# Sums of two weight matrices in the attention loop: from 16 on ScalarE in a row to 8 on ScalarE and 8 on VectorE, one of each in five units

## The chip, the core and the metric

The kernel runs on one core of a Trainium2 chip. A core has five engines that run side by side, each its own instruction list in order: TensorE (PE, matrix products and transposes, with a weight load of its own, PEld), VectorE (DVE), ScalarE (ACT), GpSimd (POOL) and SyncE (SP, which here only starts transfers). They wait for each other by semaphores written out in the program. The metric is the device time of one execution in microseconds (us); lower is better.

## What is computed

```python
# q, k, v: (2, 8, 768, 64); n_global = 8, n_local = 96
scores = q @ k^T / 8 + bias            # bias falls with the distance, by head
keep   = (key < n_global) | (0 <= query - key < n_local)
a      = softmax(where(keep, scores, -1e9));  x = a @ v      # -> (1536, 512)
h      = x @ w_in                      # (512, 2048)
x2     = (h * tanh(softplus(h))) @ w_out                     # (2048, 512)
p      = domain_probs / sum            # (1536, 4)
y      = sum over 4 experts e of p[:, e] * (relu(x2 @ w1[e]) @ w2[e])
```

## The kernel before, in words

**Stages.** First the attention, for 16 heads (two batches of eight), then the product with w_in, its activation and the product with w_out (48 steps T), then four experts. The large products run in f16, with each f32 operand split into a high and a low part and three products of them. To split a matrix it is first scaled by a power of two found from a bound on its values. For w_in and w_out this bound is a maximum over partial sums of absolute values; the change is about these.

**The attention loop.** Heads go in pairs (PAIRS = 8). A pair has UNITS = 12 units: six tiles of 128 queries by two heads. So there are 96 units; unit n is pair n // 12, place n % 12. Only the keys of the band are taken: 128 at places 0 and 1, 256 at 2 and 3, 288 at the others. For a unit the work goes round between engines: PE makes scores (line 547, for two units at a time, at odd places, three units ahead), DVE adds the bias and finds the maximum (line 1120, two units ahead), ACT takes the exponential (line 850, two units ahead), PE transposes (line 579), ACT copies the high part of the result (line 891), DVE makes the low part (line 1231), PE multiplies with the values (line 598, two units behind). Three score buffers and two buffers of transposed weights tie these together. At places 0, 2, 4, 6 PE transposes q and k of the next pair into PSUM bank 3 (fill, line 502), which ACT copies out one place later (lines 840, 843). DVE divides and stores half a pair at places 8 to 10 and 1 to 3 (output, its large step, line 1160, at 10 and 3). In pair 0 ACT also sums three pieces of v (line 874, units 2, 4, 6) and DVE reduces others (line 1201).

**The sums.** w_in lies in the tile stage, w_out raw in wB, each in eight pieces of 128 x 1024. `weights_sum(n, c)` (line 861 on) is one ACT instruction that sums the absolute values of a piece into a column of wpieces. W_SUMS places them at the end of ACT's units 21 to 28 (w_in) and 33 to 40 (w_out). DVE's `weights_max(n)` (W_MAX, units 29 and 41) reduces the columns, PE's `share_max(n)` (W_SHARE, units 32 and 44) spreads the result over the partitions by a product into bank 3, and DVE's `matrix_scale` (line 1172, W_SCALE, units 34 and 46) reads it and makes the scale in four short instructions (lines 1060 to 1063), then releases w_scale (line 1174). As bank 3 is also that of the fills, the first fill of pairs 4 and 5 waits for w_scale.

**What the scales release.** POOL waits for w_scale 1, splits w_in in eight pieces of three instructions (lines 771, 774, 777), waits for w_scale 2, and splits w_out in the same way. SP starts the loads of the first experts' w1 and w2 into stage when w_in is split (w_split 1).

**The x turns.** X0_BANDED gives the units at which PE transposes one of four chunks of the finished output of pairs 0 to 3 (line 510, bank 3), ACT copies its high part at the next unit (line 928), and DVE makes the low part at the end of its unit after that (line 1216, x_ready): units 56, 68, 80, 87. PE's turn c waits for x_ready c. From place 9 of the last pair on (unit 93) PE also makes the first products with w_in (`EARLY`); the first waits for x_ready 4 and w_split 1.

**The next stage.** By step T: PE first product (line 608), ACT exponential (line 973), DVE lines 1347, 1349, 1353, ACT lines 989 and 991, DVE lines 1365, 1367, POOL line 816, ACT line 983, DVE line 1359, and six steps behind PE's product with w_out (line 677), which waits for w_split 2. From T = 6 on DVE reduces pieces of w1 and w2 (line 1070).

Of the kernel before, what the change touches and what calls it, by code (L numbers as in the profile page):

```python
# [36 lines left out]
def program(nc, q, k, v, n_global, n_local, w_in, w_out, probs, w1, w2, out):  # L37
# [13 lines left out]
    UNITS = 2 * QT  # L51
# [21 lines left out]
    with ExitStack() as ctx:  # L73
# [166 lines left out]
        w_piece, w_sum = sem("w_piece"), sem("w_sum")  # L240
        w_max = sem("w_max")
# [71 lines left out]
        X0_BANDED = [m * UNITS + 8 for m in range(PAIRS - 4, PAIRS - 1)] + [(PAIRS - 1) * UNITS + 3]  # L313
# [12 lines left out]
        W_SUMS = ({0: 21, 1: 33}, {0: UNITS})  # L326
        W_MAX = ({n: at + PIECES for n, at in W_SUMS[0].items()}, {0: UNITS + PIECES})
        W_SHARE = ({0: 2 * UNITS + 8, 1: 3 * UNITS + 8}, {0: UNITS + 9})
# [156 lines left out]
        def _(pe):  # L485
            def fill(i, slot, k, banded):
# [9 lines left out]
                if banded and k == 0 and isinstance(m, int):  # L496
                    if m in (4, 5):
                        pe.wait_ge(w_scale, m - 3)
                    if m >= PAIRS - 2:
                        pe.wait_ge(x_ready, m - PAIRS + 3)  # L500
# [331 lines left out]
        def _(act):  # L832
# [27 lines left out]
            def weights_sum(n, c):  # L860
# [3 lines left out]
                act.wait_ge(w_sum, PIECES * n + c + len(V_SUMS))  # L864
# [18 lines left out]
            def pair(i, slot, banded):  # L883
                for u in range(UNITS):
# [19 lines left out]
                    for n, start in W_SUMS[0 if banded else 1].items():  # L904
                        if at - start in range(PIECES):
                            if n and at == start:
                                act.wait_ge(w_max, n)
                            weights_sum(n, at - start)
# [6 lines left out]
                if not banded and not after(i, slot):  # L915
                    act.wait_ge(tables_free, 1)
                    load_w_out()
                    act.wait_ge(w_max, 1)
                    for c in range(PIECES):
                        weights_sum(1, c)  # L920
# [97 lines left out]
        def _(dve):  # L1018
# [53 lines left out]

            def weights_max(n):

                halves = 1 if n < 2 else 2
                if n < 2:
                    dve.wait_ge(w_sum, PIECES * (n + 1) + len(V_SUMS))
                else:
                    dve.wait_ge(w_piece, PIECES * (n - 1))
                dve.tensor_reduce(wpart[:, 0:halves], wpieces[:].rearrange("p (h c) -> p h c", h=halves),  # L1080
# [95 lines left out]
            def matrix_step(m, u, banded):  # L1176


                at, case = m * UNITS + u, 0 if banded else 1
                for n, col in ((0, SC_WIN), (1, SC_WOUT)):  # L1180
# [254 lines left out]
            with dve.Else():  # L1435
                full_tables(chain(table_step))
                attention(False)
                dve.sem_inc(tables_free, 1)
                weights_max(1)
# [26 lines left out]
```

## Time and profile before

| | us |
|---|---|
| median of 3 runs | 910.69 (910.62 to 911.55) |
| the profiled execution | 911.57 |
| its span in the profile | 909.7 |
| attention, first to last line 1231 | 16.2 to 150.0 |

The profile counts from the start of the span. An engine is busy while one of its instructions runs; register, branch and semaphore instructions don't count. Matmuls are pipelined and their ends are modelled. A row of the timeline gives start and length, and in brackets how long the engine was idle before and which instruction released it. A row of busy times by stretch gives, behind the stretch and its length, the busy time of each engine in it with the number of its instructions, and then the clock that was granted to TensorE as a part of 2.4 GHz.

### The profile page before, as it was taken

How to read it: one execution, taken by the hardware profiler on the slowest of the kernel's cores; microseconds unless marked ns; L12 is line 12 of the kernel's file. 1: busy time of each engine (PE TensorE's matmuls, PEld its weight loads, DVE VectorE, ACT ScalarE, POOL GpSimd, SP SyncE). 2: the span in 40 equal slices, each digit the busy share in tenths (PEclk: the TensorE clock that was granted, in tenths of full speed). 3: DMA queues.
4: the chain of work that ended last, by engine and by line, in shares of the span. 5: the costliest groups of instructions: out<-in, count | busy, mean ns of one | idle time of the engine just before them, and what ended most of it. 6: DMA issues, size and time to landing. Idle time of an engine off the chain costs nothing.

```text
span 909.7 us, 12637 instructions
## 1 busy us (share of the span) xinstructions
PE 874.2 (96%) x4916; PEld 443.7 (49%) x4916; DVE 501.0 (55%) x1010; ACT 316.3 (35%) x597; POOL 263.6 (29%) x218
## 2 busy tenths in 40 slices
PE   6878999899999999999999999999999999999998
PEld 6666776444444444444444444444444444444443
DVE  7665887999999999984641224322134322212121
ACT  4798886544554555463020111101020101101020
POOL 1368993222222232220009400068000193000000
PEclk9898999999999999999999999999999999999999
DMA  9771320000000000202000400000400000000001
GB/s 222 244 251 39 124 99 1 1 1 1 1 7 3 1 1 1 93 3 93 4 6 0 180 6 1 6 0 8 177 1 2 4 0 0 1 24 23 35 12 49
DMA packets 52004, 39.19 MB, mean 43 GB/s; under 512 B 40816, under 2 KB 41712, under 8 KB 51440
## 3 DMA queue, kind: packets, MB, share of 16 engines
q1 hardware_dynamic: 49888, 34.31, 12.6%
q10 hardware_dynamic: 2064, 4.19, 1.3%
q8 instruction: 31, 0.51, 0.2%
q14 instruction: 21, 0.17, 0.1%
HBM read 35.35 MB, written 3.15 MB: 42 GB/s over the span
## 4 chain that ended last, share of the span: by engine, by line
PE 70%; DVE 20%; ACT 7%; issue 2%; POOL 0%; DVEq 0%; ACTq 0%
PE bank L608 58%; PE bank L677 5%; DVE tmp L1349 4%; DVE tmp L1367 3%; DVE xT L1365 3%; PE bank L547 2%; DVE tmp L1347 2%; PE bank L579 2%; ACT scaled L866 2%; DVE tmp L1353 2%; PE bank L598 2%; DVE hid L1359 1%; ACT tmp L989 1%; ACT tmp L850 1%; ACT tmp L891 1%
## 5 line engine op out<-in xcount | busy, mean ns | idle before, releaser
L962 ACT ACTIVATE hid<-bank 128x512 f16<-128x512 f32 x96 | 57.2, 596 | 413.8 <-PE bank L608 413.8
L608 PE MATMUL bank<-xT,wA 128*128 128x512 f16 (+1 forms) x864 | 194.6, 379 | 0.0
L1340 DVE SCALAR_TENSOR_TENSOR hid<-bank,hid 128x512 f16<-128x512 f32 x96 | 66.3, 691 | 177.2 <-ACT hid L962 177.2
L677 PE MATMUL bank<-hid,wB 128*128 128x512 f16 x576 | 133.8, 383 | 5.4 <-ACT acc L946 4.2
L608 PEld LDWEIGHTS bank<-xT,wA 128*128 128x128 f16 x864 | 84.5, 98 | 100.7 <-issue 0.2
L608 PE MATMUL bank<-wA,hid 128*128 128x512 f16 x576 | 125.3, 379 | 0.0
L608 PE MATMUL bank<-wB,hid 128*128 128x512 f16 x576 | 125.3, 379 | 0.0
L608 PE MATMUL bank<-xT,wB 128*128 x576 | 125.3, 379 | 0.0
L816 POOL TENSOR_TENSOR tmp<-tmp 128x512 f32<-128x512 f32 x48 | 67.8, 1412 | 195.8 <-DVE tmp L1367 195.8
L771 POOL TENSOR_SCALAR stage<-stage,sc 128x1024 f32<-128x1024 f32 x32 | 35.8, 1120 | 255.1 <-DVEq L1333 245.3
L1418 DVE SCALAR_TENSOR_TENSOR acc<-bank,pg,acc 128x512 f32<-128x512 f32 x36 | 27.0, 751 | 131.7 <-PE bank L608 131.7
L677 PEld LDWEIGHTS bank<-hid,wB 128*128 128x128 f16 x576 | 56.6, 99 | 75.2 <-DVE hid L1359 5.2
L608 PEld LDWEIGHTS bank<-wB,hid 128*128 128x128 f16 x576 | 56.4, 98 | 68.0
L608 PEld LDWEIGHTS bank<-xT,wB 128*128 128x128 f16 x576 | 56.4, 98 | 68.0
L608 PEld LDWEIGHTS bank<-wA,hid 128*128 128x128 f16 x576 | 56.3, 98 | 68.0
L983 ACT ACTIVATE hid<-tmp 128x512 f16<-128x512 f32 x48 | 30.3, 630 | 116.5 <-POOL tmp L816 116.5
L1231 DVE SCALAR_TENSOR_TENSOR tmp<-bank,tmp 128x384 f16<-128x384 f32 (+2 forms) x96 | 47.0, 490 | 34.2 <-ACT tmp L891 33.1
L608 PE MATMUL bank<-xT,hid 128*128 (+1 forms) x288 | 63.6, 379 | 0.0
L579 PE MATMUL bank<-ident,tmp 128*128 128x128 f32 x240 | 45.7, 290 | 8.7 <-DVE tmp L1231 6.6
L850 ACT ACTIVATE tmp<-tmp 128x288 f32<-128x288 f32 (+2 forms) x96 | 48.6, 507 | 15.5 <-DVE tmp L1120 14.4
L1349 DVE SCALAR_TENSOR_TENSOR tmp<-tmp 128x512 f32<-128x512 f32 x48 | 52.1, 1086 | 1.6
L608 PEld LDWEIGHTS bank<-xT,hid 128*128 128x128 f16 x288 | 28.2, 98 | 34.0
(111 smaller groups left out, 940.8 us busy)
## 6 DMA issues: line engine op xcount, KB each, us to landing
stage<-in_moe_w SPq DMA_DIRECT2D x8, 2048.0 KB, 9.9
stage<-in_moe_w_in SPq DMA_DIRECT2D x1, 4096.0 KB, 14.5
wB<-in_moe_w_out ACTq DMA_DIRECT2D x1, 4096.0 KB, 15.9
hid<-in_q SPq DMA_DIRECT2D x16, 192.0 KB, 3.3
hid<-in_k SPq DMA_DIRECT2D x16, 192.0 KB, 3.4
xT<-in_v SPq DMA_DIRECT2D x8, 384.0 KB, 4.9
out_y<-acc SPq DMA_DIRECT2D x12, 256.0 KB, 2.0
rows<-max SPq DMA_DIRECT2D x4, 128.0 KB, 3.8
```

The source lines that it names most:

```text
L579: last = pe.transpose(dst[:, b * P:(b + 1) * P], src[:, b * P:(b + 1) * P], ident[:])
L608: last = pe.matmul(dst, lhs(c, a), rhs(c, b), start=(c == 0 and n == 0), stop=(c == chunks - 1 and n == 2))
L677: last = pe.matmul(psum(4 + d), w_out_s[:, a, f // 2, f % 2, d * P:(d + 1) * P], hv[:, T % RING, b, :], start=(f == 0 and n == 0), stop=(f ...
L771: pool.tensor_scalar(tmp, src, scale, 1.0, ALU.mult, ALU.mult).then_inc(w_part, 1)
L816: pool.tensor_tensor(g_t[T % 4], g_t[T % 4], r_t[T % 2], ALU.mult).then_inc(g_ready, 1)
L850: act.activation(t, t, ACT.Exp, bias=nmax[:, u:u + 1], scale=-1.0).then_inc(p_ready, 1)
L962: act.activation(hv[:, f, 0, :], psum(f % 4), ACT.Relu).then_inc(f_hi, 1)
L983: act.activation(hv[:, m % RING, 0, :], g_t[m % 4], ACT.Copy).then_inc(h_hi, 1)
L1231: dve.scalar_tensor_tensor(pt[:, 1], src, P_SCALE, pt[:, 0], ALU.mult, ALU.subtract).then_inc(pT_dve, 1)
L1340: dve.scalar_tensor_tensor(hv[:, f, 1, :], psum(f % 4), 0.0, hv[:, f, 0, :], ALU.max, ALU.subtract).then_inc(f_ready, 1)
L1349: dve.scalar_tensor_tensor(n, u, 2.0, u, ALU.add, ALU.mult).then_inc(n_ready, 1)
L1365: dve.scalar_tensor_tensor(e_t, n, 2.0, r, ALU.add, ALU.mult).then_inc(e_ready, 1)
```

## The change

The pieces are dealt out: pieces 0 to 3 of each matrix to ACT (`BY_ACT`), 4 to 7 to DVE (`BY_DVE`), by a new function `weights_part_sum`, one tensor_reduce for the maximum of the absolute values of a piece into a column of wpieces. ACT's stand at the ends of units 22, 27, 32, 37 (w_in) and 46, 51, 56, 61 (w_out), DVE's in units 24, 29, 34, 39 and 48, 53, 58, 63. ACT's first sum of w_out now waits for the maximum over those of w_in, DVE's too. The maxima are taken in units 43 and 67, shared in 44 and 68, the scales made in 46 and 70. Fills of pairs 5 and 7 wait for w_scale. The x turns move to units 80, 85, 88, 90; the fills' waits for x_ready go. The branch for a mask that is no band changes in the same way; it isn't run with these inputs.

```diff
@@ -310,7 +311,7 @@
-        X0_BANDED = [m * UNITS + 8 for m in range(PAIRS - 4, PAIRS - 1)] + [(PAIRS - 1) * UNITS + 3]
+        X0_BANDED = [(PAIRS - 2) * UNITS + 8] + [(PAIRS - 1) * UNITS + u for u in (1, 4, 6)]
@@ -323,9 +324,13 @@
-        W_SUMS = ({0: 21, 1: 33}, {0: UNITS})
-        W_MAX = ({n: at + PIECES for n, at in W_SUMS[0].items()}, {0: UNITS + PIECES})
-        W_SHARE = ({0: 2 * UNITS + 8, 1: 3 * UNITS + 8}, {0: UNITS + 9})
+        BY_ACT, BY_DVE = range(4), [(4,), (5,), (6,), (7,)]
+        PARTS = len(BY_ACT) + len(BY_DVE)
+        W_ACT = ([2 * UNITS - 2 + 5 * c for c in BY_ACT], [4 * UNITS - 2 + 5 * c for c in BY_ACT])
+        W_DVE = ([2 * UNITS + 5 * c for c in range(len(BY_DVE))], [4 * UNITS + 5 * c for c in range(len(BY_DVE))])
+        W_ACT_FULL, W_DVE_FULL = ([UNITS + c for c in BY_ACT], [UNITS + c for c in range(len(BY_DVE))])
+        W_MAX = ({0: 3 * UNITS + 7, 1: 5 * UNITS + 7}, {0: UNITS + 8})
+        W_SHARE = ({0: 3 * UNITS + 8, 1: 5 * UNITS + 8}, {0: UNITS + 9})
@@ -494,10 +499,8 @@
-                    if m in (4, 5):
-                        pe.wait_ge(w_scale, m - 3)
-                    if m >= PAIRS - 2:
-                        pe.wait_ge(x_ready, m - PAIRS + 3)
+                    if m in (5, 7):
+                        pe.wait_ge(w_scale, (m - 3) // 2)
@@ -861,7 +864,9 @@
                 if c == 0:
                     act.wait_ge(w_out_loaded if n else w_loaded, 16)
-                act.wait_ge(w_sum, PIECES * n + c + len(V_SUMS))
+                    if n:
+                        act.wait_ge(w_max, n)
+                act.wait_ge(w_sum, len(BY_ACT) * n + c + len(V_SUMS))
@@ -1070,14 +1073,26 @@
+            def weights_part_sum(n, c):
+
+                if c == 0:
+                    dve.wait_ge(w_out_loaded if n else w_loaded, 16)
+                    if n:
+                        dve.wait_ge(w_max, n)
+                src = w_out_raw if n else stage
+                m, at = BY_DVE[c][0], len(BY_ACT) + c
+                dve.tensor_reduce(wpieces[:, at:at + 1], src[:, m * PIECE:(m + 1) * PIECE], AX_X, ALU.max,
+                                  apply_absolute_value=True).then_inc(w_part_sum, 1)
+
             def weights_max(n):
 
-                halves = 1 if n < 2 else 2
                 if n < 2:
-                    dve.wait_ge(w_sum, PIECES * (n + 1) + len(V_SUMS))
-                else:
-                    dve.wait_ge(w_piece, PIECES * (n - 1))
+                    dve.wait_ge(w_sum, len(BY_ACT) * (n + 1) + len(V_SUMS))
+                    dve.wait_ge(w_part_sum, len(BY_DVE) * (n + 1))
+                    dve.tensor_reduce(wpart[:, 0:1], wpieces[:, 0:PARTS], AX_X, ALU.max).then_inc(w_max, 1)
+                    return
@@ -1177,6 +1192,10 @@
                 at, case = m * UNITS + u, 0 if banded else 1
+                for n in range(2 if banded else 1):
+                    units = W_DVE[n] if banded else W_DVE_FULL
+                    if at in units:
+                        weights_part_sum(n, units.index(at))
```

## Rows read from the trace of the kernel before

**Rows 1.** Page, part 1: busy us (share of the span) and instructions of each engine.
```profile
PE 874.2 (96%) x4916; PEld 443.7 (49%) x4916; DVE 501.0 (55%) x1010; ACT 316.3 (35%) x597; POOL 263.6 (29%) x218
```

**Rows 2.** Busy time by stretch: stretch, its length, busy us by engine, granted clock, DMA.
```profile
core 0: us, PE busy (x) PEld busy (x) DVE busy (x) ACT busy (x) POOL busy (x), PEclk, DMA share, GB/s
47.93:84.71 36.78, 27.28 (x299) 21.99 (x298) 20.32 (x83) 35.44 (x82) 25.27 (x29) 0.91 0.45 138
88.11:113.84 25.73, 24.00 (x309) 19.92 (x306) 20.88 (x83) 20.85 (x51) 24.60 (x19) 1.00 0.40 122
```

**Rows 3.** Line 1231: instructions, ns min/median/max, first and last start us.
```profile
L1231 DVE SCALAR_TENSOR_TENSOR tmp<-bank,tmp x96: 275/556/559, 16.2 to 150.0; 128x384 f16<-128x384 f32 x64, 128x128 f16<-128x128 f32 x16, 128x256 f16<-128x256 f32 x16
```

**Rows 4.** Busy time by stretch: units 46, 10, 68-69, 44-45, 70.
```profile
89.27:91.60 2.33, 2.15 (x28) 1.46 (x27) 2.04 (x8) 0.63 (x2) 2.16 (x3) 1.00 0.07 15
33.24:34.38 1.14, 0.92 (x4) 0.54 (x4) 1.14 (x7) 0.78 (x2) 0.00 (x0) 0.50 0.92 374
116.31:118.78 2.47, 2.47 (x35) 2.00 (x35) 1.83 (x9) 2.31 (x6) 2.30 (x3) 1.00 1.05 402
87.19:89.27 2.08, 2.08 (x32) 1.64 (x30) 1.75 (x9) 1.92 (x5) 2.08 (x2) 1.00 1.04 232
118.78:120.52 1.74, 1.27 (x23) 0.83 (x22) 1.74 (x6) 0.63 (x2) 1.71 (x1) 1.00 0.45 159
```

**Rows 5.** Lines 866, 874 (ACT), 1201, 1070 (DVE): ns min/median/max, first and last start.
```profile
L866 ACT ACTIVATE scaled<-stage x8: 1042/1057/1096, 48.5 to 61.4; 128x1024 f32<-128x1024 f32 x8
...
L874 ACT ACTIVATE scaled<-xT x3: 827/830/831, 18.7 to 25.7; 128x768 f32<-128x768 f32 x3
...
L1201 DVE TENSOR_REDUCE vpart<-xT x4: 941/943/952, 14.2 to 23.9; 128x1 f32<-128x768 f32 x4
...
L1070 DVE TENSOR_REDUCE wpieces<-stage x32: 1208/1210/1220, 185.3 to 695.7; 128x1 f32<-128x1024 f32 x32
```

**Rows 6.** Busy time by stretch: units 1-6, 61-66, then 11-13 and 47-49.
```profile
16.70:27.04 10.34, 9.02 (x95) 7.71 (x95) 7.53 (x24) 8.93 (x22) 0.00 (x0) 0.83 0.98 223
107.79:114.79 7.00, 6.98 (x90) 6.00 (x86) 5.76 (x21) 6.73 (x15) 6.56 (x6) 1.00 0.91 341
34.38:39.93 5.55, 5.55 (x53) 4.67 (x52) 2.44 (x12) 2.73 (x8) 1.47 (x2) 0.57 1.01 411
91.60:94.69 3.09, 2.13 (x26) 1.82 (x26) 2.42 (x13) 2.63 (x8) 3.07 (x2) 1.00 0.02 5
```

**Rows 7.** Timeline of pair 7, PE, ACT, DVE: start us, length us, instruction.
```profile
141.24 0.52 PE L579 MATMUL bank<-ident,tmp 128*128 128x128 f32 x3
...
142.34 0.52 PE L579 MATMUL bank<-ident,tmp 128*128 128x128 f32 x3 [0.31 <-DVE tmp L1231]
...
144.38 0.52 PE L579 MATMUL bank<-ident,tmp 128*128 128x128 f32 x3
...
145.37 1.46 PE L608 MATMUL bank<-xT,wA 128*128 128x512 f16 x6
...
141.12 0.49 ACT L891 ACTIVATE tmp<-bank 128x384 f16<-128x384 f32 x1
...
142.11 0.68 DVE L1216 TENSOR_TENSOR xT<-bank,xT 128x512 f16<-128x512 f32 x1
```

**Rows 8.** Releases after the scales (line 1174), and POOL's last piece, from the timeline.
```profile
L1174 DVEq EVENT_SEMAPHORE  x2: 21/21/21, 71.2 to 90.8; - x2
...
141.19 2.14 POOL L777 TENSOR_TENSOR wB<-scaled,wB 128x1024 f16<-128x1024 f32 x1
```

**Rows 9.** Next stage: timeline of lines 1347, 816, 1349; then lines 1349, 677.
```profile
153.61 0.43 DVE L1347 TENSOR_SCALAR tmp<-tmp 128x512 f32<-128x512 f32 x1 [0.81 <-ACT tmp L973]
...
164.78 1.38 POOL L816 TENSOR_TENSOR tmp<-tmp 128x512 f32<-128x512 f32 x1 [4.83 <-DVE tmp L1367]
...
165.07 1.64 DVE L1349 SCALAR_TENSOR_TENSOR tmp<-tmp 128x512 f32<-128x512 f32 x1
...
L1349 DVE SCALAR_TENSOR_TENSOR tmp<-tmp x48: 691/693/1644, 154.1 to 395.4; 128x512 f32<-128x512 f32 x48
...
L677 PE MATMUL bank<-hid,wB x576: 376/379/634, 172.0 to 424.1; 128*128 128x512 f16 x192
```

More of the change, by code:

```diff
@@ L240, in program @@
         w_piece, w_sum = sem("w_piece"), sem("w_sum")
+        w_part_sum = sem("w_part_sum")
         w_max = sem("w_max")
@@ L903, in pair @@
                         load_w_out()
[L904 to L908, printed above, removed]
+                    for n in range(2 if banded else 1):
+                        units = W_ACT[n] if banded else W_ACT_FULL
+                        if at in units:
+                            weights_sum(n, units.index(at))
                     if at + 1 in V_SUMS:
@@ L917, in pair @@
                     load_w_out()
-                    act.wait_ge(w_max, 1)
-                    for c in range(PIECES):
+                    for c in BY_ACT:
                         weights_sum(1, c)
@@ L1071, in weights_part @@
                                   apply_absolute_value=True).then_inc(w_piece, 1)
+            def weights_part_sum(n, c):
[7 more added lines that the diff above has]
+                                  apply_absolute_value=True).then_inc(w_part_sum, 1)
             def weights_max(n):
-                halves = 1 if n < 2 else 2
                 if n < 2:
-                    dve.wait_ge(w_sum, PIECES * (n + 1) + len(V_SUMS))
-                else:
-                    dve.wait_ge(w_piece, PIECES * (n - 1))
-                dve.tensor_reduce(wpart[:, 0:halves], wpieces[:].rearrange("p (h c) -> p h c", h=halves),
+                    dve.wait_ge(w_sum, len(BY_ACT) * (n + 1) + len(V_SUMS))
+                    dve.wait_ge(w_part_sum, len(BY_DVE) * (n + 1))
+                    dve.tensor_reduce(wpart[:, 0:1], wpieces[:, 0:PARTS], AX_X, ALU.max).then_inc(w_max, 1)
+                    return
+                dve.wait_ge(w_piece, PIECES * (n - 1))
+                dve.tensor_reduce(wpart[:, 0:2], wpieces[:].rearrange("p (h c) -> p h c", h=2),
                                   AX_X, ALU.max).then_inc(w_max, 1)
@@ L1179, in matrix_step @@
                 at, case = m * UNITS + u, 0 if banded else 1
+                for n in range(2 if banded else 1):
+                    units = W_DVE[n] if banded else W_DVE_FULL
+                    if at in units:
+                        weights_part_sum(n, units.index(at))
                 for n, col in ((0, SC_WIN), (1, SC_WOUT)):
@@ L1438, in _ @@
                 dve.sem_inc(tables_free, 1)
+                for c in range(len(BY_DVE)):
+                    weights_part_sum(1, c)
                 weights_max(1)
```

## The prediction

> **What bounds the kernel now.** I read the head of the page first [rows 1]: TensorE (PE) is busy 96% of the 909.7 us span, VectorE (DVE) 55%, ScalarE (ACT) 35%. That is an average. The change touches only the banded attention, some 17% of the span, and there the busy shares by stretch are what counts [rows 2]. I cut this stage at the starts of the DVE instruction of line 1231, which runs once in each of the 96 units, in order [rows 3]; so a unit's length is the distance between two of them. "Unit 46" is pair 3, place 10.
>
> Two stretches with the same places in them (place 9 of one pair to place 6 of the pair after next, 21 units) are to be set side by side [rows 2]. Units 21 to 41, in which ACT makes all 16 sums of the weights, take 36.78 us: ACT is busy 35.44 of them, PE 27.28. Units 45 to 65 take 25.73 us with PE busy 24.00, DVE and ACT 20.9 each. So ACT bounds the loop while it sums; without the sums PE does, with DVE and ACT about 19% idle. A loop of short steps handed from PE to ACT to DVE and back can use little of that idleness at one time: this is the question of the whole case.
>
> **What is removed.** Units 45 to 65 hold one scale and one x turn, which I price by single units [rows 4]. The scale: unit 46 took 2.33 us, unit 10, at the same place and with the same work in the loop, 1.14; so 1.19 (unit 10 ran at the low clock, so rather more). The x turn: units 68 and 69 took 2.47, units 44 and 45 took 2.08, and unit 70 took 1.74 against 1.14; so 0.39 + 0.60 = 0.99. Without both the 21 units take 25.73 - 1.19 - 0.99 = 23.55 us. The 16 sums of before, with the scale of |w_in| that fell among them (unit 34) and was mostly hidden, therefore cost 36.78 - 23.55 = 13.2 us, 0.8 each against the 1.04 to 1.06 that one takes on ACT [rows 5]. All of this goes.
>
> **What is added: eight sums on ACT and eight on DVE.** On DVE no such sum stands in the attention. The same instruction on 1024 columns takes 1.21 us later in the kernel, and one on 768 columns takes 0.94 us in pair 0; ACT's on 768 takes 0.83 [rows 5]. From below: in 21 units DVE has 25.73 - 20.88 = 4.85 us free, 1.15 in five units, and ACT 1.16. Both sums would then fit, and cost 0 to 0.3 us for both (below nothing is excluded, since both engines only get more work). From above: each passes on whole, 1.04 + 1.21 = 2.25 us. In between lies the one place where the two kinds alternate: units 1 to 6 hold three ACT and three DVE sums of 768 columns and took 10.34 us, against 7.00 for the same places in units 61 to 66 [rows 6]. That is 3.34 us for three pairs, 1.11 for a pair that occupies 0.83 + 0.94 us, so 0.63 per us of work; for 2.25 us it gives 1.4. The clock was down for a part of it and the sums stood closer than five units apart, both of which make it high; the DVE sums at places 3 and 10 now sit beside the output step, where the scale, a few short DVE instructions, cost 1.19, which makes it low. I take 1.3. Eight pairs: 8 x 1.3 = 10.4 us (0 to 18.0).
>
> **The scales.** The scale of |w_in| moves from unit 34, where ACT hid most of it, to unit 46; that of |w_out| from 46 to 70. Each now stands in the open: 2 x 1.19, where before one was inside the 13.2. The one at 46 was in the time before already, so +1.2 us more.
>
> **The x turns.** There are four before and after, now at units 80, 85, 88 and 90 in place of 56, 68, 80 and 87: 4 x 0.99 either way. But turn 3 (unit 90) waits for the low half of turn 2, which DVE makes only at the end of its unit 90, and the first product in unit 93 waits for the low half of turn 3, at the end of DVE's unit 92. PE is in order: behind the wait are turn 91, the scores and the values. By the rows of pair 7 [rows 7]: the transposes of unit 90 start at 141.24 and end at 141.76, then come ACT's copy (0.49), line 1231 (0.56), line 1216 (0.68) and the steps between, to about 143.6, and 0.3 of transposes; unit 91's transposes start at 143.9 and not at 142.34, 1.6 later, of which 1.0 is in the price of a turn. At unit 93 the same chain runs from 144.90 to about 146.8, where the first product started at 145.37: 1.4 later, of which 0.6 is priced. Together +1.4 us (0 if PE's other waits cover it, 3.0 if nothing of it is in the price of a turn).
>
> The two waits of PE for x_ready at fills of pairs 6 and 7 go; they waited for nothing (no row). The wait of ACT for w_max at unit 46 stands three units behind its release: nothing.
>
> **GpSimd (POOL), behind both scales.** It splits |w_in| from the first scale on: released at 71.2, its last piece of w_out starts at 141.19 and takes 2.14 [rows 8], so it ends at 143.3, 72.1 us after the release, and is never idle between. The second scale came at 90.8, long before POOL wanted it, which is at half way, 36 us on. Now it comes at unit 70. From unit 46 to 70 it was 118.78 - 89.27 = 29.5 us [rows 4]; less two x turns (2.0) and with four pairs of sums (5.2) that is 32.7, still before POOL is ready for it. So POOL ends 72.1 us after the scale of unit 46. The first DVE instruction of the next stage, line 1347, started at 153.61 [rows 9], 62.8 us after that same point of before (90.8). Now this distance grows by four pairs of sums (5.2), the second scale (1.2) and the x turns' waits (1.4) to 70.6. POOL's last piece would thus run 1.5 us into the next stage. What this costs is shown by line 1349: 1.64 us when it starts behind a POOL tensor_tensor at 164.78, where its median is 0.69 and POOL's instruction takes 1.38 [rows 9]. So DVE's lines 1347 and 1349 wait for POOL, and they are where the chain runs (ACT and PE wait for their result). I take +1.5 us (0 to 2.1). The products with w_out start only at 172.0 [rows 9]; POOL ends at about 155, so PE doesn't wait for it. The loads of w1 and w2 start behind w_in's split, 11.6 us later; the first reader of them stands at 185.3 [rows 5], so nothing.
>
> The Trainium skill ("SBUF — State Buffer", "Who interferes with whom") says that DVE with two SBUF inputs, or in a two-port mode, blocks against GpSimd for whole instructions, and that tensor_reduce never does. The trace agrees: 1.64 against 0.69 us for the one, 1208 to 1220 ns in all 32 cases for the other. By the rule the new DVE sums don't slow down beside POOL's splits, and the tail above is real.
>
> **The sum.** -13.2 + 10.4 + 1.2 + 1.4 + 1.5 = +1.3 us. Against the profiled execution (911.57 us, with 909.7 of span) that is 912.9; against the median of 910.69, **912.0 us**. What comes behind the attention is the same work in the same order, so the difference is handed through whole.
>
> **The rivals.**
> Rival A, the sums are absorbed. With the idle 19% of DVE and ACT used, a pair costs 0 to 0.3. For it: the busy shares, and that ACT and DVE are loaded in turn, not one engine in every unit. Against it: units 1 to 6. Then the scale of unit 46 comes at 90.8 - 13.2 + 1.0 = 78.6; POOL ends 72.1 later, at 150.7, and the next stage would begin 62.8 + 1.0 + 1.2 + 1.4 = 66.4 later, at 145.0. If DVE's first lines wait for POOL to the last, the end comes 2.9 us earlier than before, if never, 8.6: 902.1 to 907.8, and as each wait is for one POOL instruction of three, about the middle, 905.5 us. Faster.
> Rival B, every sum is passed on whole (2.25 a pair), since a unit is a ring of PE, ACT and DVE with two buffers. For it: DVE's 0.68 us of line 1216 made unit 70 0.60 longer. Against it: 0.8 each even where ACT was the bound. -13.2 + 18.0 + 1.2 + 1.4 + 0 (POOL is done by then) = +7.4: 918.1 us. Slower; it decides from 1.4 us a pair on.
> Rival C, the clock. Among ACT's 16 sums the granted clock fell from 2.4 to 1.2 GHz for a while (mean 0.91 [rows 2]), behind a stretch in which PE was busy for 27.28 of 36.78 us; there it was covered, as ACT was the bound. In the open it isn't: units 11 to 13, up to unit 14, took 5.55 us at a mean of 0.57, units 47 to 49, up to unit 50, which are the same places, 3.09 at 1.00 [rows 6]. The sums now stand in the open with PE idle beside them, so one such spell costs 2.5 on top of the sum: 914.5 us. Slower.
> Rival D, the waits of the x turns and of POOL's tail aren't there: -13.2 + 10.4 + 1.2 = -1.6: 909.1 us, no difference to speak of. That the change doesn't do what it says can hardly be: the banded branch is the one in the trace.
>
> **How the numbers follow.** About 0.2%, 1.8 us, is what a measurement of this kernel can tell from no change, so "same" is 908.9 to 912.5. The sum as worked has 0.45; its terms move it by 1.5 either way, and a part of 0.12 lies above 912.5. Rival A 0.25, B 0.13, C 0.13, D 0.04. Faster 0.25; same 0.33 + 0.04 = 0.37; slower 0.12 + 0.13 + 0.13 = 0.38. The range leaves out the lower part of A and what lies past B: 904.5 to 918.0; the forecast alone is 910.5 to 913.5.
>
> **What would show it.** In the profile after: the distance of line 1231 over units 21 to 45 falls by about 8 us; single units with an ACT sum are 0.5 to 0.8 longer, with a DVE sum 0.5 at places 0 and 5 and about 1.1 at 3 and 10; PE waits for line 1216 ahead of unit 91 and ahead of the first product; POOL's last piece ends behind the first line 1347, which takes over 1 us. The forecast is wrong if the units with sums are no longer than their neighbours (A), if each is 1 us longer (B), or if the clock is low between units 22 and 66 (C).

## The result, and the profile after

The changed kernel takes 914.2 us (median of 7 runs, 912.56 to 914.89) against 910.62 for the kernel before (7 runs, 909.53 to 911.56): ratio 1.0039, 95% interval 1.0029 to 1.0049. Measured again, unaltered, on another chip it took 913.93 against 911.33: 1.0031 (1.0022 to 1.0041). So it is slower by 0.3 to 0.4%, about 3 us. The time forecast was 912.0, in a range of 904.5 to 918.0; the side on which it came out had a chance of 0.38.

The head of the page after: the span, the busy shares (as [rows 1]), and the granted clock in 40 slices.

```profile
span 912.3 us, 12632 instructions
...
PE 873.6 (96%) x4916; PEld 443.0 (49%) x4916; DVE 510.5 (56%) x1018; ACT 308.5 (34%) x581; POOL 263.8 (29%) x218
...
PEclk8899999999999999999999999999999999999999
```

The shares of the whole span say nothing: PE is at 96% as before. So I cut the attention as in the forecast, at the starts of the DVE instruction that makes the low part (line 1231 before, 1250 after). The stretches are units 21 to 45, 46 to 83, 84 to 92, 93 and 94, and from unit 95 to the next stage's first tensor_scalar (line 1347 before, 1366 after). Columns are those of [rows 2]: stretch, length, busy us of PE, PEld, DVE, ACT, POOL, clock, DMA. First the kernel after:

```profile
47.15:81.22 34.07, 28.40 (x361) 23.29 (x359) 27.08 (x95) 27.87 (x67) 12.27 (x18) 1.00 0.59 174
81.22:132.36 51.14, 42.94 (x547) 35.23 (x546) 41.63 (x148) 40.50 (x97) 47.30 (x34) 1.00 0.30 99
132.36:146.44 14.08, 10.03 (x123) 8.42 (x124) 10.01 (x35) 8.99 (x21) 13.27 (x10) 1.00 0.01 2
146.44:150.80 4.36, 4.36 (x40) 2.69 (x39) 1.68 (x6) 1.52 (x3) 4.09 (x4) 1.00 0.02 4
150.80:155.95 5.15, 5.15 (x57) 3.69 (x56) 3.20 (x6) 0.72 (x2) 3.96 (x3) 1.00 0.00 0
```

and the same five stretches of the kernel before, which [rows 2] cut elsewhere:

```profile
47.93:89.27 41.34, 31.84 (x363) 25.84 (x361) 23.93 (x98) 39.57 (x91) 29.66 (x32) 0.92 0.48 141
89.27:135.68 46.41, 42.93 (x553) 35.55 (x552) 37.98 (x140) 37.76 (x91) 44.02 (x32) 1.00 0.33 110
135.68:146.38 10.70, 9.68 (x118) 8.07 (x118) 8.80 (x35) 8.05 (x19) 7.29 (x5) 1.00 0.01 3
146.38:149.96 3.58, 3.58 (x37) 2.30 (x35) 1.67 (x7) 1.52 (x3) 0.00 (x0) 1.00 0.00 0
149.96:153.61 3.65, 3.65 (x46) 2.55 (x45) 1.70 (x7) 0.72 (x2) 0.00 (x0) 1.00 0.00 0
```

| stretch | before | after | difference |
|---|---|---|---|
| up to unit 21 | 47.93 | 47.15 | -0.78 |
| units 21 to 45 | 41.34 | 34.07 | -7.27 |
| units 46 to 83 | 46.41 | 51.14 | +4.73 |
| units 84 to 92 | 10.70 | 14.08 | +3.38 |
| units 93, 94 | 3.58 | 4.36 | +0.78 |
| unit 95 to the next stage | 3.65 | 5.15 | +1.50 |
| the rest of the span | 756.09 | 756.35 | +0.26 |
| sum, the span | 909.7 | 912.3 | +2.6 |

The first line is not the change: nothing is altered up there, and 0.70 of the 0.78 us lie ahead of the first unit. Nor is the last but one: the 48 steps of the next stage start at the same distances in both (the last at 241.39 us behind the first, and at 241.37), and the 0.26 comes behind them. The five lines between are the change: it costs 3.1 us, where the medians show 3.6 and 2.6. Outside stretches of low clock the length of a unit repeats from one execution to the next to some 0.02 us, so these differences are far sharper than the medians.

**Single units with a sum.** Kernel after, busy time by stretch: units 22 (an ACT sum, place 10), 24 (DVE, place 0), 27 (ACT, 3), 29 (DVE, 5) and 34 (DVE, 10).

```profile
48.21:49.91 1.70, 1.70 (x27) 1.24 (x26) 1.23 (x4) 1.70 (x5) 1.49 (x4) 1.00 1.03 324
50.73:52.40 1.67, 1.63 (x23) 1.42 (x22) 1.67 (x7) 0.67 (x2) 1.59 (x2) 1.00 1.08 383
54.98:57.30 2.32, 2.32 (x31) 2.04 (x27) 1.26 (x4) 2.32 (x6) 2.16 (x4) 1.00 1.08 388
58.15:60.12 1.97, 1.42 (x17) 1.04 (x16) 1.97 (x7) 1.28 (x3) 1.89 (x2) 1.00 0.57 134
65.14:67.41 2.27, 2.27 (x30) 1.57 (x30) 2.27 (x6) 0.89 (x2) 0.00 (x0) 1.00 0.06 13
```

The same places without a sum took 1.14 (place 10, [rows 4]), 0.82, 1.44, 1.43 and 1.14 us in the kernel before. So the sums cost 0.56, 0.85, 0.88, 0.54 and 1.13 us in their own units. In the units with a DVE sum DVE is busy for the whole of the unit and ACT for a good third to two thirds of it; in those with an ACT sum ACT is busy for the whole and DVE for half to three quarters. Over all 25 units (which take 28.11 us without a sum: the 23.55 us of the forecast's 21 units, and 4.56 for units 42 to 45) the four pairs cost 34.07 - 28.11 = 5.96 us, 1.49 a pair. In units 46 to 83 two x turns (2.0) went and a scale (1.2) came; 4.73 + 2.0 - 1.2 = 5.5, 1.38 a pair.

**The x turns.** Timeline of PE in the kernel after: the transposes of turns 2 and 3 (line 513) and the first product with w_in (line 611).

```profile
137.69 0.66 PE L513 MATMUL bank<-ident,acc 128*128 128x128 f32 x4 [1.31 <-DVE xT L1235]
...
141.87 0.66 PE L513 MATMUL bank<-ident,acc 128*128 128x128 f32 x4 [1.50 <-DVE xT L1235]
...
146.21 1.04 PE L611 MATMUL bank<-xT,wA 128*128 128x512 f16 x4 [1.20 <-DVE xT L1235]
```

In brackets stands PE's idle time before each: 1.31, 1.50 and 1.20 us, ended each time by DVE's line 1235 (1216 before), which makes the low half of the turn ahead. The transposes of unit 91 waited 0.31 us in [rows 7], for another line, and the first product not at all.

**POOL's tail.** Kernel after: the releases behind the two scales (line 1189, as 1174 in [rows 8]), POOL's last instruction of w_out, then the next stage's first DVE instructions.

```profile
L1189 DVEq EVENT_SEMAPHORE  x2: 21/21/21, 82.8 to 116.4; - x2
...
152.80 2.13 POOL L780 TENSOR_TENSOR wB<-scaled,wB 128x1024 f16<-128x1024 f32 x1
...
153.30 1.65 DVE L1334 TENSOR_TENSOR sc<-sc 128x1 f32<-128x1 f32 x1
154.98 0.16 DVE L1335 TENSOR_TENSOR sc<-sc 128x1 f32<-128x1 f32 x1
155.95 0.43 DVE L1366 TENSOR_SCALAR tmp<-tmp 128x512 f32<-128x512 f32 x1 [0.81 <-ACT tmp L976]
```

POOL is released at 82.8 and ends at 154.93, 72.1 us later, as in the kernel before. Line 1334 is a product of two columns of 128x1. The one like it in the kernel before took 0.15 us; here it starts 0.50 us behind the start of POOL's tensor_tensor and ends 0.02 us behind its end, 1.65 us long. All of the 1.50 us by which the stretch from unit 95 on grew are in this one instruction. The first tensor_scalar of the stage starts at 155.95, 1.0 us behind POOL's end.

### The profile page after: what moved, and what is told of

It is laid out like the page before. It is cut to its first block, busy times and chain, and to the rows that moved or that the text cites. A ratio compares the mean times of both kernels' runs of the same rounds, so it can differ in the third digit from the quotient of the medians.

```text
span 912.3 us, 12632 instructions
## 1 busy us (share of the span) xinstructions
PE 873.6 (96%) x4916; PEld 443.0 (49%) x4916; DVE 510.5 (56%) x1018; ACT 308.5 (34%) x581; POOL 263.8 (29%) x218
## 4 chain that ended last, share of the span: by engine, by line
PE 68%; DVE 22%; ACT 6%; issue 2%; SPq 1%; DMA 0%; POOL 0%; DVEq 0%; ACTq 0%
PE bank L611 58%; PE bank L680 5%; DVE tmp L1368 4%; DVE tmp L1386 3%; DVE xT L1384 3%; DVE tmp L1366 2%; PE bank L550 2%; DVE tmp L1372 2%; PE bank L582 1%; DVE hid L1378 1%; ACT tmp L896 1%; ACT tmp L992 1%; PE bank L601 1%; ACT tmp L853 1%; DVE tmp L1135 1%
## 5 line engine op out<-in xcount | busy, mean ns | idle before, releaser
L1250 DVE SCALAR_TENSOR_TENSOR tmp<-bank,tmp 128x384 f16<-128x384 f32 (+2 forms) x96 | 47.0, 489 | 28.4 <-ACT tmp L896 27.4
L896 ACT ACTIVATE tmp<-bank 128x384 f16<-128x384 f32 (+2 forms) x96 | 41.4, 431 | 11.1 <-PE bank L582 10.4
```

The costliest lines, as they stand in the source:

```text
L896: act.activation(pt[:, 0], src, ACT.Copy, scale=P_SCALE).then_inc(pT_act, 1)
L1250: dve.scalar_tensor_tensor(pt[:, 1], src, P_SCALE, pt[:, 0], ALU.mult, ALU.subtract).then_inc(pT_dve, 1)
```

## The experiments

Ratios are to the kernel before on the same chip; where I say what a run has gained on the changed kernel "by the ratios", the changed kernel stands at 1.0035, the mean of its two. With a clock that falls at different moments, the median of a dozen runs is good to about 1 us (of the version in 9 there are only six and five); where a trace has the answer to 0.1 us, I go by the trace and give the median beside it.

**1. x turns that don't wait for each other.**

```diff
-        X0_BANDED = [(PAIRS - 2) * UNITS + 8] + [(PAIRS - 1) * UNITS + u for u in (1, 4, 6)]
+        X0_BANDED = [4 * UNITS + 8, 6 * UNITS + 8, 7 * UNITS, 7 * UNITS + 4]
...
                         pe.wait_ge(w_scale, (m - 3) // 2)
+                    if m == 6:
+                        pe.wait_ge(x_ready, 1)
```

> The changed kernel with the x turns at units 56, 80, 84 and 88, so that no turn and no first product waits for the low half of the turn before. Theory 1 (the loss comes from PE's three waits for line 1235 in pair 7, 2.2 us beyond the price of the turns, and from POOL's tail, which ends 72.05 us after the first scale whatever the loop does): the waits go and the last unit of the loop comes 2.2 us earlier, but POOL still ends at about 154.9, so DVE's first instructions of the next stage wait for POOL 1.5 to 3 us and most of the gain is given back: 912.5 to 914 us, against 914.2 for the changed kernel. Theory 2 (PE's waits cost, POOL's tail does not): 912.0. Theory 3 (it is the sums alone, the waits are covered): 914.2.

Measured: 911.62 us, ratio 1.0012 (0.9998 to 1.0025), 2.1 us under the changed kernel by the ratios. Busy time by stretch: units 84 to 92, 93 and 94, and from unit 95 to the next stage.

```profile
137.68:148.21 10.53, 9.73 (x118) 7.97 (x119) 9.24 (x36) 8.45 (x20) 9.91 (x8) 1.00 0.01 2
148.21:151.90 3.69, 3.69 (x37) 2.37 (x36) 1.67 (x6) 1.52 (x3) 3.42 (x4) 1.00 0.02 4
151.90:155.96 4.06, 4.06 (x50) 2.96 (x49) 2.10 (x7) 0.72 (x2) 3.87 (x3) 1.00 0.00 0
```

Units 84 to 92 take 10.53 us against 14.08, units 93 and 94 3.69 against 4.36: 4.2 us less, of which 1.1 came back as the turn at units 57 and 58 of this kernel, so 3.1 us. That is more than the 2.2 that I had set down as waits. The units around the two turns at 84 and 88 take 10.53 us, less than in the kernel before with one turn, at 87 (10.70): in pair 7, where there are no fills, a turn that nothing waits for seems to cost less than the 1.0 among the fills, though no run has pair 7 without a turn.

POOL took a part of this back. Its last instruction, and DVE's small product and first scalar_tensor_tensor of the next stage:

```profile
156.16 2.21 POOL L782 TENSOR_TENSOR wB<-scaled,wB 128x1024 f16<-128x1024 f32 x1
...
154.40 0.55 DVE L1336 TENSOR_TENSOR sc<-sc 128x1 f32<-128x1 f32 x1
156.42 2.50 DVE L1370 SCALAR_TENSOR_TENSOR tmp<-tmp 128x512 f32<-128x512 f32 x1
```

POOL ends at 158.37, 2.4 us into the next stage. The small product took 0.40 us longer than in the kernel before (0.15), and the scalar_tensor_tensor 1.81 longer than the 0.69 that it takes in the changed kernel; the second step of the stage starts 3.60 us behind the first in place of 1.80. So POOL's tail costs 2.2 us here against 1.5, and 2.4 of the 3.1 us are left, near the 2.1 of the ratios. Theory 1, by which most of the gain would be given back, was wrong in size: about a quarter was.

**2. POOL shorter.** The first of the eight pieces of w_out is set to zero in place of being split.

```diff
                 hi, lo = (wB[:, (2 * c + s) * PIECE:(2 * c + s + 1) * PIECE] for s in range(2))
+                if c == 0:
+                    pool.memset(wB[:, 0:2 * PIECE], 0.0).then_inc(w_out_part, 1)
+                    continue
```

> The changed kernel with the first of the eight pieces of w_out not split by POOL but set to zero by one memset (this part of w_out is left out of the result), so that POOL ends about 3.5 us earlier; nothing else is touched. Theory 1: the 1.65 us of line 1334 (128x1, waiting for POOL's last tensor_tensor) fall back to 0.15, and the kernel takes 914.2 - 1.5 = 912.7 us. Theory 2 and 3 (POOL's tail is covered): 914.2, with line 1334 short and the time lost elsewhere.

Measured: 912.15 us, ratio 1.0014 (1.0001 to 1.0027). Timeline of POOL's last instruction and of the small product:

```profile
150.05 2.13 POOL L780 TENSOR_TENSOR wB<-scaled,wB 128x1024 f16<-128x1024 f32 x1
...
153.39 0.15 DVE L1337 TENSOR_TENSOR sc<-sc 128x1 f32<-128x1 f32 x1
```

POOL ends at 152.18, ahead of it, and the product takes 0.15 us. Unit 95 to the next stage is 3.65 us again, as in the kernel before: exactly the 1.50 are gone. Units 84 to 94 stayed as long as in the changed kernel (18.4 us). Theory 1 holds for this term, to 0.1 us in the trace; the ratios give 1.9 us.

**3. Both.** The two edits together.

> Both at once: x turns at 56, 80, 84, 88 and POOL's first piece of w_out left out (set to zero). Theory 1: the two losses add up once POOL is out of the way: 914.2 - 2.2 - 1.5 = 910.5 us, so that the turns apart are worth 2.2 us here and much less in the run where POOL stays long. Theory 2: 912.0. Theory 3: 914.2.

Measured: 911.55 us, ratio 1.0019 (1.0007 to 1.0032). By the medians this is a miss: no faster than either alone. In the trace the span was 907.4, units 84 to 92 took 10.53 and 93 and 94 3.70 us, as in run 1. But the loop was now so much shorter that the small product met POOL all the same (1.95 us long, a tail of 1.8 us), so this run did not take the tail away, and says nothing on whether the two add up. Its single runs went from 909.25 to 915.7, over 6.4 us; only run 1 (6.3) and the second measurement of run 4 (6.4) spread as far. More on this stands at the end, under the clock.

**4. The kernel before with the late turns.** Run twice.

```diff
-        X0_BANDED = [m * UNITS + 8 for m in range(PAIRS - 4, PAIRS - 1)] + [(PAIRS - 1) * UNITS + 3]
+        X0_BANDED = [(PAIRS - 2) * UNITS + 8] + [(PAIRS - 1) * UNITS + u for u in (1, 4, 6)]
...
-                    if m >= PAIRS - 2:
-                        pe.wait_ge(x_ready, m - PAIRS + 3)
```

> The kernel before with only the x turns moved to units 80, 85, 88 and 90; sums, scales and POOL as before (POOL ends some 10 us ahead of the next stage). Theory 1 and 2: PE waits for the low halves ahead of turns 2 and 3 and ahead of the first product, +2.2 us: 910.6 + 2.2 = 912.8 us. Theory 3: 910.6.

> The kernel before with only the x turns moved to 80, 85, 88 and 90, once more. Its trace showed the units 84 to 93 longer by 3.37 us (two more turns at 1.0 each and 1.4 of waits) and unit 93 by 0.78, so 2.1 us net, while its median was only 0.3 us above the kernel before, with 4.8 us less of low clock in its runs on average. If the 2.1 us are real and the clock hid them by chance: 911.5 to 912.9 here. If the later turns make the clock fall less often, which gives them back: the median stays within 0.8 us of the kernel before and the mean time at the low clock is again about 5 us shorter.

Measured: 910.61 us, 1.0003 (0.9994 to 1.0013), and again 911.62 us, 1.0011 (0.9997 to 1.0025). Busy time by stretch of the second, as in run 1:

```profile
132.46:146.53 14.07, 10.02 (x123) 8.42 (x123) 10.01 (x35) 8.97 (x21) 9.28 (x7) 1.00 0.00 1
146.53:150.89 4.36, 4.36 (x40) 2.69 (x39) 1.68 (x6) 1.51 (x3) 0.00 (x0) 1.00 0.01 4
150.89:154.54 3.65, 3.65 (x46) 2.55 (x45) 1.69 (x6) 0.72 (x2) 0.00 (x0) 1.00 0.00 0
```

Units 84 to 92 take 14.07 us and units 93 and 94 4.36, in both executions, the lengths of the changed kernel to 0.01; the last stretch is 3.65, since POOL is done. From unit 21 to the next stage both traces show 107.7 us against 105.7 before: +2.0. So the waits are made by the places of the turns alone. The medians show less, 0.3 and 1.0 us. The traces show where the rest may be. Behind the attention, too, both executions were shorter than the kernel before, by 1.70 us each, and it is all in one place: a group of 48 products with w_out. Busy time by stretch from the start of the 385th of them to that of the 433rd, kernel before and then the first of these two:

```profile
342.34:364.74 22.40, 22.40 (x96) 9.83 (x97) 21.65 (x29) 12.72 (x22) 6.56 (x5) 0.92 0.00 1
...
342.25:362.97 20.72, 20.72 (x97) 9.40 (x98) 19.97 (x28) 12.16 (x20) 5.49 (x5) 1.00 0.00 1
```

A fall of the clock there, which the profiled execution of the kernel before had and these two had not, costs 1.7 us. It hides most of the 2.0 us in these traces; how often it comes in the other runs, nothing here shows. By each run's mean granted clock, the runs of this kernel spent 21.8 and 24.1 us at the low clock on average, against 25.4 and 27.4 for the kernel before on the same chips. Whether the later turns are what makes the clock fall less often, or chance, these runs don't settle.

**5 and 6. DVE's sums left out, ahead of the first scale and behind it.** Run 5 leaves out the four DVE sums of w_in, run 6 those of w_out; the bound is taken over ACT's pieces alone. The edit of run 5 is shown; run 6 has n != 1 in its place.

```diff
-                    if at in units:
+                    if at in units and n != 0:
                         weights_part_sum(n, units.index(at))
```

> The changed kernel without DVE's four sums of w_in (units 24, 29, 34, 39; the maximum is taken over ACT's four, so half of w_in is left out of its bound). They stand ahead of the first scale. Theory 1 (POOL is the bound from the first scale on): they cost 0.85 + 0.7 + 1.1 + 0.9 = 3.5 us, and as the scale and with it POOL come earlier by that, the whole of it is gained: 914.2 - 3.5 = 910.7 us. Rival (the loop is the bound to its end): the same 3.5.

> The changed kernel without DVE's four sums of w_out (units 48, 53, 58, 63; half of w_out is left out of its bound). They stand behind the first scale. Theory 1: the loop ends 3.4 us earlier, POOL does not, and DVE's first two-input instructions of the next stage wait for POOL's last pieces: 913 to 914 us. Rival (the loop is the bound, POOL's tail costs what it costs): 914.2 - 3.4 = 910.8, as with the sums of w_in left out.

Measured: run 5 910.86 us, 0.9997 (0.9988 to 1.0007); run 6 911.65 us, 1.0007 (0.9997 to 1.0017). Against the changed kernel that is 3.5 and 2.5 us less by the ratios. Run 5 is as expected; run 6 is not: theory 1 gave it 0.2 to 1.2 us, the rival 3.4. The timeline of run 6 shows why: POOL's last instruction, then DVE's small product, the first tensor_scalar and scalar_tensor_tensor of the next stage, and the second tensor_scalar.

```profile
153.41 2.44 POOL L780 TENSOR_TENSOR wB<-scaled,wB 128x1024 f16<-128x1024 f32 x1
...
150.54 0.41 DVE L1336 TENSOR_TENSOR sc<-sc 128x1 f32<-128x1 f32 x1
151.96 0.47 DVE L1368 TENSOR_SCALAR tmp<-tmp 128x512 f32<-128x512 f32 x1 [0.81 <-ACT tmp L976]
152.47 1.40 DVE L1370 SCALAR_TENSOR_TENSOR tmp<-tmp 128x512 f32<-128x512 f32 x1
154.51 1.63 DVE L1368 TENSOR_SCALAR tmp<-tmp 128x512 f32<-128x512 f32 x1
```

The stage began at 151.96, and POOL ended at 155.85, 3.9 us later. DVE did not wait for that end. It lost 0.26 us on the small product, 0.71 on the scalar_tensor_tensor at 152.47 and 1.2 on the tensor_scalar at 154.51, 2.2 us together, and went on between POOL's instructions. With POOL's end as a bound DVE would have lost 4.2 us: without a wait the stage would have begun at 151.70. So POOL's tail is a toll and not a bound: 1.5 us where one instruction meets it, 2.2 (run 1) and 2.7 (run 7, below) where it reaches 2.4 us into the stage, and 2.2 here, at 3.9. This refutes theory 1 in its strong form, and agrees with run 1, where most of the gain stayed.

**7. Both sums in one unit.**

```diff
-        W_DVE = ([2 * UNITS + 5 * c for c in range(len(BY_DVE))], [4 * UNITS + 5 * c for c in range(len(BY_DVE))])
+        W_DVE = W_ACT
```

> The changed kernel with DVE's sums in the same units as ACT's (22, 27, 32, 37 and 46, 51, 56, 61) and not two units behind. If the loop is held by the ring of PE, ACT and DVE, two stops at the same time cost about one: a pair of sums costs 1.1 to 1.2 us in place of 1.43. Four pairs ahead of the first scale move the end by 1.0 to 1.3 us, the four behind it nothing, as POOL is the bound there: 913.0. If stops add up wherever they stand: 914.2.

Measured: 911.63 us, 1.0005 (0.9994 to 1.0016), 2.7 us under the changed kernel by the ratios. Busy time by stretch: units 21 to 45, then 22, 27 and 32, each with both sums.

```profile
47.16:78.89 31.73, 27.85 (x361) 23.10 (x359) 27.21 (x95) 28.37 (x67) 13.29 (x20) 1.00 0.63 185
48.22:50.49 2.27, 2.09 (x29) 1.39 (x27) 2.27 (x6) 1.67 (x4) 2.11 (x4) 1.00 0.99 337
54.44:56.82 2.38, 1.74 (x23) 1.40 (x19) 2.38 (x6) 2.35 (x5) 2.21 (x3) 1.00 1.08 391
61.57:63.62 2.05, 1.52 (x26) 1.25 (x25) 2.05 (x6) 1.81 (x4) 0.11 (x2) 1.00 0.75 171
```

A unit with both sums is 0.94 to 1.13 us longer than a plain one, and the 25 units take 31.73 us: (31.73 - 28.11) / 4 = 0.91 a pair, against 1.49 two units apart. Run 5, with ACT's sums alone, gives the price of each kind over the same units:

```profile
47.89:78.61 30.72, 27.81 (x361) 22.97 (x359) 22.96 (x91) 28.25 (x67) 12.35 (x18) 1.00 0.65 193
```

ACT's four sums cost 30.72 - 28.11 = 2.61 us, 0.65 each, and DVE's four in the changed kernel 34.07 - 30.72 = 3.35, 0.84 each. Two units apart the two prices add up (1.49); in one unit the pair costs little more than DVE's sum alone. DVE's sums also stand at other places of the pair here, which could be a cause of its own; but pairs in one unit at still other places cost the same in run 9. The gain was larger than expected, since the pairs behind the first scale gained too: units 21 to 94 took 99.7 us against 103.7, and POOL's tail, 2.7 us, took only 1.2 more than in the changed kernel.

**8. A version: sums in a row on both engines.** The changed kernel with the shares, scales, turns and PE's waits of the kernel before, and:

```diff
-        W_ACT = ([2 * UNITS - 2 + 5 * c for c in BY_ACT], [4 * UNITS - 2 + 5 * c for c in BY_ACT])
+        W_ACT = ([21 + c for c in BY_ACT], [33 + c for c in BY_ACT])
+        W_DVE = W_ACT
...
+        W_MAX = ({0: 25, 1: 37}, {0: UNITS + 8})
```

> A version: ACT and DVE each sum four pieces in a row in the same units, 21 to 24 (w_in) and 33 to 36 (w_out); maxima at 25 and 37; scales at 34 and 46 and x turns at 56, 68, 80 and 87 as in the kernel before, so that POOL ends long ahead of the next stage. A unit with both sums should be held by DVE and be about 1.05 us longer: 8 x 1.05 = 8.4 us for all sums, where the 16 in a row on ACT took 13.2 with the first scale in it; the first scale now stands in the open, +0.8. So -4.0: 906.6 us. If stops of ACT and DVE add up as in the changed kernel (1.43 for two sums): -13.2 + 11.4 + 1.2 = -0.6, 910.0.

Measured: 910.28 us, 0.9989 (0.998 to 0.9997). The forecast of the sums was right, that of the time was not. Busy time by stretch: units 21 to 24, with the sums, and 25 to 28 behind them.

```profile
47.59:55.75 8.16, 5.05 (x65) 3.89 (x63) 7.90 (x21) 7.03 (x17) 7.42 (x12) 0.97 1.04 359
55.75:62.75 7.00, 6.12 (x43) 4.95 (x40) 3.95 (x16) 4.42 (x11) 5.04 (x8) 0.55 0.65 199
```

Units 21 to 24 took 8.16 us against 3.9 plain, 1.05 to 1.1 more for a unit with both sums, as expected. In them PE was busy for 5.05 of 8.16 us. Then the granted clock fell to 1.2 GHz for most of the next four units: 7.00 us at a mean of 0.55, against 4.6 for the same places at 2.4 GHz. Behind the sums of w_out it fell again, 0.7 us. So 3.1 of the 4.0 us went to the clock; from unit 21 to 95 the trace has 101.0 us against 102.0 before. That the time came out near the 910.0 of the rival, in which the two kinds of sums add up, is chance. The Trainium skill ("TensorE: Matmul & The Clock Gate", "Part 1: The HAM clock gate (the 'warmup' mystery)") says that an idle TensorE is set back to half its clock; here it was busy for 62% of the four units before the fall, with pauses between, and not idle all along, so this run shows a fall that the sentence alone doesn't cover.

**9. A version: both sums in one unit, some units apart, the first scale early.** Run twice.

```diff
-        W_ACT = ([2 * UNITS - 2 + 5 * c for c in BY_ACT], [4 * UNITS - 2 + 5 * c for c in BY_ACT])
+        W_ACT = ([21, 24, 27, 30], [37, 42, 47, 52])
+        W_DVE = W_ACT
...
+        X0_BANDED = [5 * UNITS + 8, 6 * UNITS + 8, 7 * UNITS, 7 * UNITS + 4]
...
+        W_MAX = ({0: 31, 1: 54}, {0: UNITS + 8})
+        W_SHARE = ({0: 2 * UNITS + 8, 1: 4 * UNITS + 8}, {0: UNITS + 9})
...
+                    if m in (4, 6):
+                        pe.wait_ge(w_scale, (m - 2) // 2)
+                    if m == 7:
+                        pe.wait_ge(x_ready, 1)
```

> A version: ACT and DVE sum a piece each in the same unit, at units 21, 24, 27, 30 (w_in) and 37, 42, 47, 52 (w_out); first scale at 34 as in the kernel before, second at 58, so that POOL, which needs it 36 us after the first, ends long ahead of the next stage; x turns at 68, 80, 84 and 88, where none waits for another. By unit lengths of the run with both sums in one unit: 8 pairs x 1.0 = 8 us for the sums, two scales in the open 2.4, four turns as before: -13.2 - 1.2 + 8.0 + 2.4 = -4.0, so 906.7 us if the clock is as in the kernel before. The rival is the clock: sums only three units apart leave PE idle for 1 us in 3.3, and if that brings a stretch of 6.8 us at 1.2 GHz in the open behind them, as behind the sums in a row, 2.5 us of it are lost: 909.2.

> The version with both sums in one unit at 21, 24, 27, 30 and 37, 42, 47, 52, scales at 34 and 58 and x turns at 68, 80, 84 and 88 once more, since its first measurement rests on few runs. If its 0.9934 (0.9913 to 0.9955) was not luck of the clock: a ratio of 0.992 to 0.995, 904 to 907 us, and the same unit lengths in its trace (96.3 us from unit 21 to 95, against 102.0 for the kernel before). If stretches of low clock fall among its sums in other executions: above 0.996, with single runs near 909.

Measured: 905.2 us, 0.9934 (0.9913 to 0.9955), and again 904.38 us, 0.9931 (0.9917 to 0.9945). It beats both kernels, by 6 us and 9 us. Busy time by stretch of the first: units 21 to 45, 84 to 92, 93 and 94, and on to the next stage.

```profile
47.01:81.64 34.63, 28.47 (x361) 23.36 (x359) 30.11 (x102) 29.84 (x71) 27.18 (x30) 1.00 0.58 173
129.11:139.64 10.53, 9.74 (x118) 7.98 (x118) 9.24 (x36) 8.46 (x20) 9.53 (x7) 1.00 0.01 2
139.64:143.33 3.69, 3.69 (x37) 2.37 (x36) 1.67 (x7) 1.52 (x3) 0.00 (x0) 1.00 0.02 4
143.33:146.98 3.65, 3.65 (x46) 2.55 (x45) 1.70 (x6) 0.72 (x2) 0.00 (x0) 1.00 0.00 0
```

In the first stretch there are six pairs of sums and a scale (1.19) over 28.11 us: 34.63 - 29.30 = 5.33, 0.89 a pair. The clock stays at 1.00 throughout. No turn waits (10.53 and 3.69 us), POOL ends at 139.18, and the last stretch is 3.65. From unit 21 to 95 it is 96.3 us against 102.0 before: -5.7, in both executions. That is more than the expected -4.0 by the sums (5.33 for six pairs and 2.0 for the two in units 47 and 52, 7.4 us in place of 8.0) and by 1.0 in pair 7, where this version has two turns and the kernel before one, in the same time. The pairs stand at places 9, 0, 3, 6 and 1 in the first stretch, three units apart at first, and cost what they did in run 7, five units apart: so neither the places nor the distance to the next pair explains the low price; the common unit is what the two runs share.

**The base of the last runs.** The changed kernel was measured once more beside runs 4 and 9:

> The changed kernel once more, unaltered, on the chip of the next two runs, as their base. Expected: the same ratio as in its first measurement, 1.0039 (1.0029 to 1.0049), so about 3.5 us above the kernel before; and in the trace the same lengths of units 22 to 95 outside stretches of low clock (34.07 us from unit 21 to 46, 14.08 from 84 to 93), a pause of PE of 1.3 to 1.5 us ahead of turns 2 and 3 and of 1.2 ahead of the first product, and POOL's last piece ending 72.05 us after the first scale.

It came out at 1.0031 (above), with 34.08 us for units 21 to 45 and 14.07 for 84 to 92, PE's pauses of 1.32, 1.50 and 1.20 us, and POOL's end 72.1 us behind the release.

## Why the prediction came out as it did

- **The number.** 914.2 lies in the range, but above the 910.5 to 913.5 of the forecast alone, and next to rival C's 914.5, though the clock was at 1.00 in all five stretches. That nearness is chance: two terms below, the new sums and the turns' waits, were too low, and none was too high.
- **ACT is the bound among the 16 sums; they cost 13.2 us with the first scale.** Units 21 to 45 fell by 7.27, where the terms gave 13.2 - 5.2 = 8.0. Right, with the new sums costing 0.76 more in this stretch.
- **The new sums: 1.3 a pair.** Measured 1.49 and 1.38, 11.5 us for eight pairs and not 10.4. The place of pair 0 [rows 6] gave 1.41, and I went below it, on the grounds that the clock was low there and that a greater distance between sums helps. The second fails: 0.91 in the same unit, 1.43 two units apart, and pairs three units from each other cost no more than pairs five units apart (run 9). The term was mis-sized by 1.1 us, by correcting a row by an argument. DVE's sums at places 10 and 3 cost 1.1 and 0.9, at place 5 0.5, as forecast; at place 0, forecast at 0.5, 0.85.
- **The scales: 1.2 us more.** Unit 70 of the changed kernel took 2.33 us, as unit 46 in [rows 4]. Right.
- **The x turns: 4 x 0.99 either way, and 1.4 us of waits.** The waits ahead of turn 3 and of the first product are there. I overlooked the one ahead of turn 2 in unit 88, which waits for the low half of turn 1 that DVE makes at the end of its unit 87 (1.31 us idle). Units 84 to 94 became 4.2 us longer, where the terms gave 2.0 + 1.4. The step that failed is the list of waits, one short. Against turns that stand apart the places 85, 88 and 90 cost even more, 3.1 us (run 1).
- **POOL ends 72.1 us behind the first scale and meets the next stage: +1.5.** The 72.1 is right. The 1.5 came out to the tenth, but by luck. Without a wait the stage would have begun 71.6 us behind the scale and not 70.6, since the sums and turns after it took about 1 us more than forecast, so POOL's end reached 0.5 us past that point and not 1.5. The sign that I named did not show: the first tensor_scalar (1347, now 1366) took 0.43 us and POOL was done before it. What met POOL was the small product ahead of it (line 1334), which I had not listed; it was held for what was left of POOL's 2.13 us, and where in that instruction it falls is what makes the 1.5. In rival A I set the cost midway between POOL's end as a bound and nothing. Run 6 gives 2.2 of 4.2, so that was about right; the bound was the idea of theory 1, in the experiments.
- **What adds up.** +0.7 in units 21 to 45, +0.3 in 46 to 83, +0.8 in the turns, nothing behind: 1.8 us more than the 1.3 forecast, 3.1 in all. The waits and POOL's tail together, 3.7 us, are more than the sums won: 16 sums and a hidden scale at 13.2 became 11.5 and 1.2, a gain of 0.5.
- **The rivals.** A (absorbed) is out: the sums cost 1.43 a pair with DVE and ACT idle for a fifth of the loop. B (2.25 a pair) is out too. C, the clock, didn't strike the changed kernel (1.00 in all five stretches), but it did strike the version with the sums in a row, as its mechanism said. In D I held it possible that waits and tail weren't there; they are.

## What to carry to other kernels

In a loop where work goes round between three engines, two extra instructions on two engines can cost their full prices when they are staggered (here 1.43 to 1.49 us) and little more than the dearer one when both engines stop in the same step (0.89 to 0.91): look for what can be stopped together, not for what is spread evenly. When a step is moved later, list every instruction that waits for its result, one by one and on each in-order queue, and follow what it releases to its end; here the gain on the sums was 0.5 us, the turns' waits cost 2.2 and the engine that started later 1.5. If a row gives a price for nearly the same thing, don't talk it down.

## What the runs showed of the hardware

- A DVE instruction of 128x1 with two inputs in SBUF took 1.65 us when it started 0.50 us behind a POOL tensor_tensor of 2.13 us (1.95 us at 0.20 behind it, run 3), and 0.15 without it: what is left of POOL's instruction is what counts, not its own size. The changed kernel's four tensor_reduces on 1024 columns beside POOL's splits took 1209 to 1210 ns, and the four with POOL idle 1207 to 1210: not delayed.
- DVE is not held off to the end of POOL's series. With POOL 3.9 us into the next stage it lost 2.2 us in three waits (run 6); 2.4 us in, 2.2 in two (run 1).
- Outside stretches of low clock the length of a unit repeats to some 0.02 us between executions, chips and kernels, so that a term of 0.3 us can be read, while medians of a dozen runs differ by 1 us.
- The granted clock is a large part of what makes them differ. By the mean clock of the runs on one chip, the kernel before spent 27.4 us of an execution at 1.2 GHz on average, and the changed kernel 19.0. Where it falls decides what it costs. Among ACT's 16 sums it costs nothing: units 21 to 45 took 41.34 us in the kernel before and 41.34 and 41.32 in the two executions of run 4, with the low clock at different moments. In the 48 products of run 4 it costs 1.7 us at a mean clock of 0.92 (22.40 us in place of 20.72), and in the second execution of run 9 2.9, at 0.88 (23.60).
- Run 1's profiled execution, 4 us slower than its median, had three stretches at 1.2 GHz in the open between units 41 and 66 (unit 41 alone took 2.13 us in place of 1.22). What starts one in a given execution stays open.
